# First expert's weights split in two halves of columns, second-layer pieces waited for singly, 13 filler products

## What is computed

```python
scores = where(0 <= i - j < 64, q @ k.T / sqrt(64), -1e9)
x = (softmax(scores) @ v) as [1152, 512]
p = domain_probs / sum(domain_probs)
x = sum over e < 4 of p[:, e] * (relu(x @ w1[e]) @ w2[e])     # w1[e] 512x1024, w2[e] 1024x512
do = x @ w_skip > 0;  e = argmax(x[do] @ w_gate)              # one of 8 experts for each row
out = x;  out[do] += gate * (relu(x[do] @ u1[e]) @ u2[e])
```

## Time and profile before

| | us |
|---|---|
| median of 3 runs | 642.59 (642.39 to 642.60) |
| profiled execution | 641.48 |
| its span | 639.70 |
| TensorE busy | 625.9 (98%) |
| VectorE busy | 294.7 (46%) |
| ScalarE busy | 246.6 (39%) |
| GpSimd busy | 76.5 (12%) |

### The profile page before, as it was taken

The page is one execution under the profiler, slowest core; times in us unless marked ns, Lnnn a source line. Parts: engine busy times, 40 slices in busy tenths (PEclk is TensorE's granted clock), DMA queues, the critical chain, the costliest instruction groups (busy, mean ns, idle before and its releaser), DMA issues.

```text
span 639.7 us, 9836 instructions
## 1 busy us (share of the span) xinstructions
PE 625.9 (98%) x3494; PEld 560.5 (88%) x3495; DVE 294.7 (46%) x777; ACT 246.6 (39%) x518; POOL 76.5 (12%) x119
## 2 busy tenths in 40 slices
PE   8799999999999999999999999999999999999995
PEld 8788999898989898989898998989888888888884
DVE  5576556524512124512124434344567735671681
ACT  5765545522401013301013211322344755773682
POOL 6750000000000000000000001000011231231231
PEclk9999999999999999999999999999999999999998
DMA  8904043106999993210002331032246969594441
GB/s 284 281 21 133 33 128 102 71 1 202 227 268 231 279 261 132 84 47 0 0 0 70 102 107 60 3 129 94 99 151 204 332 232 282 175 352 104 153 156 32
DMA packets 51234, 89.99 MB, mean 141 GB/s; under 512 B 13113, under 2 KB 17721, under 8 KB 51201
## 3 DMA queue, kind: packets, MB, share of 16 engines
q1 hardware_dynamic: 47088, 82.15, 42.1%
q0 software_dynamic: 3440, 7.26, 4.5%
q10 hardware_dynamic: 672, 0.15, 0.1%
HBM read 63.88 MB, written 27.08 MB: 142 GB/s over the span
## 4 chain that ended last, share of the span: by engine, by line
PE 94%; POOL 2%; ACT 2%; DVE 1%; issue 1%; DVEq 0%; POOLq 0%; ACTq 0%
PE ps_y L1064 31%; PE ps_h L1064 29%; PE ps_y L1138 10%; PE ps_h L1138 10%; POOL w_lo_a L461 2%; PE ps_o L1021 2%; PE ps_s L985 2%; PE ps_s L1153 2%; PE ps_s L1041 1%; PE ps_h L1086 1%; PE ps_o L1118 1%; PE ps_h L973 1%; PE ps_t L1000 1%; PE ps_t L1127 1%; PE ps_t L1031 1%
## 5 line engine op out<-in xcount | busy, mean ns | idle before, releaser
L647 ACT ACTIVATE ht_hi<-ps_h 128x384 fp32r<-128x384 f32 (+1 forms) x104 | 48.5, 467 | 239.1 <-PE ps_h L1064 229.9
L1064 PE MATMUL ps_h<-xt_hi,w_hi_a 128*128 128x384 f32 (+1 forms) x400 | 130.9, 327 | 0.0
L1064 PE MATMUL ps_h<-xt_hi,w_lo_a 128*128 128x384 f32 (+1 forms) x400 | 129.4, 324 | 0.0
L1064 PE MATMUL ps_h<-xt_lo,w_hi_a 128*128 128x384 f32 (+1 forms) x400 | 129.4, 323 | 0.0
L1064 PE MATMUL ps_y<-w_hi_a,ht_hi 128*128 128x512 f32 x288 | 115.6, 402 | 0.5 <-POOL w_lo_a L461 0.5
L1064 PE MATMUL ps_y<-w_hi_a,ht_lo 128*128 128x512 f32 x288 | 112.7, 391 | 0.0
L1064 PE MATMUL ps_y<-w_lo_a,ht_hi 128*128 128x512 f32 x288 | 112.5, 391 | 0.0
L861 DVE SCALAR_TENSOR_TENSOR ht_lo<-ps_h,ht_hi 128x384 fp32r<-128x384 f32 (+1 forms) x104 | 54.7, 526 | 119.8 <-ACT ht_hi L647 119.7
L1064 PEld LDWEIGHTS ps_h<-xt_hi,w_hi_a 128*128 128x128 f32 x400 | 75.4, 188 | 0.5 <-DVE ht_lo L861 0.2
L1064 PEld LDWEIGHTS ps_h<-xt_lo,w_hi_a 128*128 128x128 f32 x400 | 75.4, 188 | 0.4
L1064 PEld LDWEIGHTS ps_h<-xt_hi,w_lo_a 128*128 128x128 f32 x400 | 75.3, 188 | 0.0
(11 more groups left out here) (155 smaller groups left out, 853.4 us busy)
## 6 DMA issues: line engine op xcount, KB each, us to landing
raw<-u SPq DMA_DIRECT2D x40, 512.0 KB, 4.0
x_sorted<-xg SPq DMA_DIRECT2D x4, 4112.0 KB, 43.2
raw<-w SPq DMA_DIRECT2D x32, 512.0 KB, 4.1
x<-u SPq DMA_DIRECT2D x24, 512.0 KB, 6.5
vt<-v SPq DMA_DIRECT2D x17, 256.0 KB, 2.9
xg<-x_sorted POOLq DMA_DIRECT2D x12, 257.0 KB
kt<-k SPq DMA_DIRECT2D x8, 384.0 KB, 4.7
x_sorted<-xg SPq DMA_DIRECT2D x1, 2313.0 KB, 41.3
```

The lines of the kernel that those rows point to most:

```text
L647: a.activation(ht_hi[:, pos, 0:P * tiles], ps_h[:, pos % 2, 0:P * tiles], ACT.Relu).then_inc(h_hi_done, 1)
L1064: ins = mm(dst, hi_lo[l], rhs_hi_lo[r], start=(first and n == 0), stop=(last and n == 2))
```

## The change

In ScalarE's prologue each w1 piece is converted only in its first 512 columns (`first_half`); the four second halves stand in a row behind the prologue's last copy into `xt_hi`. GpSimd makes the low parts of the four first halves, then of the four second halves, then of w2; the counting `w1_split` goes up only with a second half, and a new pair of semaphores counts the first halves. TensorE waits for the first halves before the dense blocks, for the second halves before block f=4 of the first chunk, and for the pieces of w2 one by one before every second term of the first tile. SyncE's four fetches of w2 now stand together, behind the loads of values 2 and keys 3. The first run of filler products has 13, not 18.

```diff
-    FILL_FIRST, FILL = 18, 2
+    FILL_FIRST, FILL = 13, 2
...
             load_keys(2)
-            weights(w2, 0, (w1_split, 0), pieces=(0, 1))
             load_values(2)
             load_keys(3)
-            weights(w2, 0, (w1_split, 0), pieces=(2, 3))
+            weights(w2, 0, (w1_split, 0))
             load_values(3)
...
+            first_lows = [(w1_half_hi_done, w1_half_split, j, w1_hi[0][:, j, :], w1_lo[0][:, j, :], (0, 1)) for j in range(KC)]
+            first_lows += [(w1_hi_done, w1_split, j, w1_hi[0][:, j, :], w1_lo[0][:, j, :], (2, 3)) for j in range(KC)]
+            first_lows += [(w2_hi_done, w2_split, j) + tuple(w[0][:, 2 * j:2 * j + 2, :].rearrange("p j d -> p (j d)")
+                                                           for w in (w2_hi, w2_lo)) + (range(QUARTERS),) for j in range(KC)]
...
+            def first_half(j):
+
+                act.wait_ge(raw_landed[j], 16)
+                copy(w1_hi[0][:, j, 0:F // 2], raw[:, j, 0:F // 2]).then_inc(w1_half_hi_done, 1)
+
...
                 if p - 2 in PROLOGUE_PIECES:
-                    weights_hi(0, PROLOGUE_PIECES.index(p - 2), 0)
+                    first_half(PROLOGUE_PIECES.index(p - 2))
+            for j in range(KC):
+                copy(w1_hi[0][:, j, F // 2:], raw[:, j, F // 2:]).then_inc(w1_hi_done, 1)
...
-                        pe.wait_ge(w1_split, e * KC + KC)
+                        pe.wait_ge(*((w1_half_split, KC) if first else (w1_split, e * KC + KC)))
...
+                        if first and c == 0 and f == FH:
+                            pe.wait_ge(w1_split, KC)
...
-                    if c == 0:
+                    if c == 0 and not first:
                         pe.wait_ge(w2_split, e * KC + KC)
...
+                            if first and c == 0 and i == 0 and f % 2 == 0:
+                                pe.wait_ge(w2_split, f // 2 + 1)
```

More of the change, by code:

```diff
@@ L257, in build_block @@
         w1_hi_done, w1_split = sem("w1_hi_done"), sem("w1_split")
+        w1_half_hi_done, w1_half_split = sem("w1_half_hi_done"), sem("w1_half_split")
         w2_hi_done, w2_split = sem("w2_hi_done"), sem("w2_split")
@@ L449, in _ @@
             pool.wait_ge(xg_clear, 2)
[L451 to L457, removed]
+            first_lows = [(w1_half_hi_done, w1_half_split, j, w1_hi[0][:, j, :], w1_lo[0][:, j, :], (0, 1)) for j in range(KC)]
+            first_lows += [(w1_hi_done, w1_split, j, w1_hi[0][:, j, :], w1_lo[0][:, j, :], (2, 3)) for j in range(KC)]
+            first_lows += [(w2_hi_done, w2_split, j) + tuple(w[0][:, 2 * j:2 * j + 2, :].rearrange("p j d -> p (j d)")
+                                                           for w in (w2_hi, w2_lo)) + (range(QUARTERS),) for j in range(KC)]
+            for hi_done, split, j, hi, lo, quarters in first_lows:
                 pool.wait_ge(hi_done, j + 1)
-                for n in range(QUARTERS):
+                for n in quarters:
                     own = slice(n * F // QUARTERS, (n + 1) * F // QUARTERS)
```

## The result

| | before | changed |
|---|---|---|
| median of 18 runs, us | 642.05 | 643.76 |
| lowest to highest | 641.47 to 643.55 | 642.43 to 645.53 |
| profiled execution, us | 641.48 | 643.17 |
| its span | 639.70 | 641.40 |

The ratio is 1.0025, 95% interval 1.0019 to 1.0031: 1.7 us slower, a quarter of a percent. The forecast was 642.8, and no change. The time lies inside the range for 8 in 10 (641.8 to 644.5), just above the forecast's own range (to 643.7), and near the slower rival.

The account below looks back on a forecast made before the run. TensorE, 98% busy, was taken as the bound. Gains of 2.30 us before the dense blocks were outweighed by the stall: f=3 +0.87, second-layer wait -0.66, so +0.2 on 642.59 gives 642.8 us; 8-in-10 range 641.8 to 644.5.

Parts of the forecast that it names:

- the slower rival: TensorE's idle stretch before block f=3 lowers its clock, adding 1.7 us: 644.5 us; chance 0.15.
- The fillers: Kernel start: five fewer filler products bring the first scores to about 6.2, gaining 0.72 us, bounds 0.7 and 1.11.
- The halves on ScalarE: Prologue: half conversions of w1 bring the last copy into xt_hi 1.1 us earlier, bounds 0.9 and 1.84.
- What the halves move: First dense blocks: later w2 fetch delays ScalarE's queue; TensorE idles about 3.15 us, block f=3 starts 0.87 us later.
- Behind f=3 I see no further stall: After block f=3: remaining w2 pieces land before ScalarE reaches them, its order then level with the old shifted by 0.9.
- rival 2: Block f=3: the roughly 3.1 us stall costs TensorE its clock, 1.7 us more, 644.5 us; chance 0.15.
- the likeliest case: Whole kernel: halves gain 2.3 us and lose it in a transfer, giving 642.8 us; chance 0.72.
- The second-layer wait: Start of the second layer: TensorE needs only the first w2 low part, not all four, so 0.66 us goes.
- Rival 1: Second-layer fetches come early enough, no new stall before f=3: 3.0 us go, 639.6 us; chance 0.08.

## Why the prediction was right or wrong

The timeline up to block f=3 was right to about 0.3 us. Part of that is luck: A came 0.31 us earlier than said and the way from A took 0.16 more, so f=3 fits better than either.

| instant | predicted | measured |
|---|---|---|
| first scores | 6.2 | 5.96 |
| A, end of the last copy into xt_hi | 23.57 | 23.26 |
| first dense product, released by xt_hi | 23.63 | 23.40 |
| landing of the first w2 piece, us | 3.6 | 3.79 |
| from A to f=3 | 8.44 | 8.60 |
| block f=3 | 32.0 | 31.86 |
| idle of TensorE before it | 3.15 | 3.03 |
| second layer | 41.0 | 42.42 |

- **The fillers.** I held the start to the landing of the query half at 6.18. It landed earlier, 4.1 us after its issue and not 4.7, at 5.58, and the scores followed the last filler without a gap, so the gain was 0.96 here. Even where the landing took 4.8 us (the run with 12 fillers beside f=3) it was in at 6.28, and the scores began at 6.77, straight behind the fillers: there too the fillers set the start. The size of this term is less certain than either bound said: in the eight profiles with 13 fillers the first scores began between 5.96 and 7.01, in the three with 18 between 6.92 and 7.66. It depends on how long the slow start lasts (last section). Over the runs the five fillers are worth 0.11%, 0.7 us.
- **The halves on ScalarE.** 0.9 to 1.84 us at A, 1.1 taken. Measured: 2.13 from A to A, less 0.96 of the fillers, is 1.17. Counted from the first scores, A stood at 18.5 before and at 17.3 in the changed kernel, and at 17.3 again in two more profiles of this prologue (12 fillers beside f=3, 18 at the start).
- **What the halves move.** Right: ScalarE stood 3.38 us ahead of its first w2 conversion (3.5 said), TensorE 3.03 ahead of f=3. Moving the conversions behind later blocks took the whole stretch away.
- **Behind f=3 I see no further stall.** This is the step that failed. There was no further stall, but the idle stretch itself had a price: the half clock for the eighteen products behind it, 1.58 us. The prediction had it as rival 2, with 1.7 us for it, 644.5 us, and a chance of 0.15. It was the case in the 12 of 18 runs with a granted clock of 0.994 or less, by its windows in the profiled one, which has 0.996, and by their times probably in the other two with 0.996. The three runs at 0.998 have 642.43 to 642.93 us, where the forecast of the likeliest case was 642.8.
- **Why the chance was too small.** The argument against it was that waits of 1.2 us leave the rate whole. That says nothing of 3 us, and a rival for which no row speaks either way should, as I judge it now, have had about half of the chance. The Trainium skill (TensorE: Matmul & The Clock Gate, HAM oscillation — how this bites in real kernels) describes this pattern, a wait for a transfer between runs of products that leaves the products behind it at the lower clock. The trace agrees in that: a granted clock of 0.50 behind a wait of 3.03 us. It differs in the moment, since that section puts the fall into the wait, and here it came just after.
- **How near the number came.** Nearer than the working deserves. The change was forecast at +0.2 us and measured at +1.7. The time is only 1.0 above the forecast because the kernel before had a median of 642.05 over 18 runs, where the three runs that the forecast starts from had 642.59. Two slips stand in the sums besides: the forecast's own range goes down by 0.4 and 0.7, to 641.7 and not 641.9, and rival 2 adds 1.7 for a slow start that the sentence before puts at 1.8.
- **The second-layer wait.** Right: 0.66 us, gone in the changed kernel and alone (the single waits).
- **Rival 1**, no stall at all, 639.6: not what this change does, but what it does with w2 converted later (ratio 0.9963 and 0.9956, 639.7 and 639.2 on the median of 642.05).

## What to carry to other kernels

When a count that releases a buffer is made to rise later, look for the transfer that it gates, then for the instruction that waits for that transfer, and then for what stands behind it in its engine's list. Here a conversion in front of a small copy turned a gain of 2.4 us or more into a loss of 1.7, and moving it behind two or three more blocks brought the gain. On TensorE an idle stretch of some microseconds is not paid once: add the slow products behind it to the price, or put filler products into it. Read the mean granted clock of every run beside its time: 0.998 and 0.994 parted runs that had paid from those that had not. In between it does not decide, because the end of the kernel counts in it.

## What the hardware showed that I had not expected

- The clock can fall after the idle stretch has ended: products began at 31.86 and the half clock shows from about 32.1 (the window 31.9 to 33.6 has 0.56); with six fillers it fell about a microsecond after the first product. With 18 fillers at the start it fell half a microsecond before the first product. So the moment is not tied to the end of the stretch.
- How long an idle stretch costs the clock is not a fixed matter: 1.8 us did in 4 of 11 runs, 3.0 us in at least 13 of 18, two of up to 1.2 us in the prologue of the kernel before showed no slow products behind them.
- The slow start of TensorE has no fixed length either. The same 26 filler instructions took 4.82 us in the profile of the changed kernel and 5.78 with the fillers alone changed:

```profile
1.31 5.78 PE L973 MATMUL ps_h<-xr 128*128 128x128 f32 x26 [1.31 <-DVE xr L915]
6.92 0.61 PE L985 MATMUL ps_s<-kt,qz 128*128 128x128 f32 x4
```

  and 36 took 5.78 before. The first scores stood at 6.92 in both. One profile of each would have shown no gain of the five fillers; the runs show 0.11%. The column of the granted clock reads 1.00 over this slow start, so only the spacing shows it.
- The first w2 piece landed after 3.6 to 3.9 us in the eight profiles with halves, the pieces behind it after 4.3 to 4.9 in most. The second piece took 6.1 us in two of the eight at the same place of the program, and 4.3 to 4.8 in the other six.
